# Splits of the output weights moved between slots of the last first-stage tile and chunks of the first second-stage tile

## The reference, cut to what matters

```python
scores  = scale * x @ state.T ; a  = softmax(scores)  ; xread = a  @ state   # 8 batches, 8 heads
scores2 = scale * state @ x.T ; a2 = softmax(scores2) ; sread = a2 @ x
x = concat([xread, sread])            # 8*512 + 8*32 = 4352 tokens, 512 features
h = relu(x @ w_in) ; x = (h*h) @ w_out        # first stage, width 2048
a = x @ w1 ; b = x @ w2                       # second stage, width 1024
out = ((a*b) @ w3) @ w_out2                   # computed as (a*b) @ (w3 @ w_out2)
```

## Time and profile before

| what | value |
|---|---|
| median of 3 runs | 1265.2 us (1264.62 to 1265.58) |
| profiled execution, its own time | 1264.61 us |
| its span, first to last instruction | 1263.0 us |
| PE busy | 1239.3 us (98%) |
| DVE busy | 809.8 us (64%) |
| ACT busy | 496.4 us (39%) |
| mean granted PE clock | 0.992 of full |

### The profile page before, as it was taken

How to read it: one execution, slowest core, us unless ns; L and a number is a source line. 1 busy time by engine, 2 the same in 40 slices (tenths; PEclk the granted TensorE clock), 3 DMA queues, 4 the chain that set the end, 5 groups by cost and what they waited for, 6 DMA issues and landing times.

```text
span 1263.0 us, 19633 instructions
## 1 busy us (share of the span) xinstructions
PE 1239.3 (98%) x7177; PEld 1081.5 (86%) x7177; DVE 809.8 (64%) x1445; ACT 496.4 (39%) x936; POOL 56.6 (4%) x101
## 2 busy tenths in 40 slices
PE   8988999999999999999999999999999999999998
PEld 5656888888888888888889989999999999999998
DVE  6665877678696866667544556575757575757541
ACT  6565565555555554445443412121212121212111
POOL 1000001111011100000000000000000000000000
PEclk9988999999999999999999999999999999999999
DMA  8986444444434322122112950101010110100210
GB/s 287 353 296 240 138 150 164 138 144 160 149 133 162 136 101 91 58 84 67 72 61 104 370 177 1 67 1 66 2 64 17 49 33 33 33 33 0 84 61 24
DMA packets 64632, 139.13 MB, mean 110 GB/s; under 512 B 5696, under 2 KB 6720, under 8 KB 64576
## 3 DMA queue, kind: packets, MB, share of 16 engines
q1 hardware_dynamic: 53984, 100.68, 23.7%
q0 software_dynamic: 10592, 37.75, 8.1%
HBM read 84.93 MB, written 53.48 MB: 110 GB/s over the span
## 4 chain that ended last, share of the span: by engine, by line
PE 95%; DMA 3%; DVE 1%; ACT 1%; issue 0%; SPq 0%; POOL 0%; DVEq 0%; ACTq 0%; POOLq 0%
PE ps_y L660 48%; PE ps_h L660 27%; PE ps_t L660 18%; DMA g_scratch<-g_extra 1%; DMA wp_scratch<-stage 1%; PE ps_h L719 1%; DMA g_scratch<-stage 1%; PE ps_t L719 1%; PE ps_t L684 0%; DMA raw<-in_moe_w_in 0%; DMA raw<-wp_scratch 0%; ACT GB L950 0%; DVE t L1203 0%; ACT v_hi L950 0%; DVE X_lo L1203 0%
## 5 line engine op out<-in xcount | busy, mean ns | idle before, releaser
L950 ACT CAST v_hi<-t 128x512 fp32r<-128x512 f32 (+1 forms) x216 | 129.1, 597 | 443.2 <-DVE t L1203 443.2
L660 PE MATMUL ps_y<-v_hi,X_hi 128*128 128x512 f32 (+1 forms) x576 | 219.6, 381 | 3.2 <-DVE stage L1292 3.2
L1203 DVE TENSOR_TENSOR v_lo<-t,v_hi 128x512 fp32r<-128x512 f32 (+1 forms) x216 | 143.0, 662 | 118.5 <-ACT v_hi L950 111.7
L660 PE MATMUL ps_y<-v_lo,X_hi 128*128 128x512 f32 (+1 forms) x576 | 218.2, 379 | 0.0
L660 PE MATMUL ps_y<-v_hi,X_lo 128*128 128x512 f32 (+1 forms) x576 | 218.0, 379 | 0.0
L1203 DVE TENSOR_TENSOR t<-t 128x256 f32<-128x256 f32 (+1 forms) x272 | 143.4, 547 | 103.2 <-ACT t L1050 100.2
L1050 ACT ACTIVATE t<-ps_h 128x512 f32<-128x512 f32 (+1 forms) x144 | 82.6, 573 | 158.8 <-PE ps_h L660 157.3
L660 PEld LDWEIGHTS ps_y<-v_hi,X_hi 128*128 128x128 f32 x576 | 108.7, 189 | 23.1 <-issue 3.7
L660 PEld LDWEIGHTS ps_y<-v_hi,X_lo 128*128 128x128 f32 x576 | 108.8, 189 | 20.4
L660 PEld LDWEIGHTS ps_y<-v_lo,X_hi 128*128 128x128 f32 x576 | 108.9, 189 | 19.4
L1203 DVE TENSOR_TENSOR t<-t,ps_t 128x256 f32<-128x256 f32 (+1 forms) x132 | 72.5, 549 | 48.4 <-PE ps_t L660 34.6
(11 more groups left out here) (235 smaller groups left out, 2816.9 us busy)
## 6 DMA issues: line engine op xcount, KB each, us to landing
raw<-g_scratch SPq DMA_DIRECT2D x64, 256.0 KB
raw<-in_moe_w_in SPq DMA_DIRECT2D x32, 256.0 KB
raw<-in_x_T SPq DMA_DIRECT2D x32, 256.0 KB
raw<-in_x_tok SPq DMA_DIRECT2D x32, 256.0 KB
y_scratch<-stage POOLq DMA_DIRECT2D x8, 1024.0 KB, 6.0
s_scratch<-top POOLq DMA_DIRECT2D x32, 256.0 KB, 2.5
s_scratch<-E_lo POOLq DMA_DIRECT2D x32, 256.0 KB, 3.7
raw<-y_scratch SPq DMA_DIRECT2D x8, 1024.0 KB, 5.3
```

Source lines behind the costliest of these rows:

```text
L660: mm = nc.tensor.matmul(dst, w, m, start=first and n == 0, stop=last and n == 2)
L950: return nc.scalar.copy(dst, src)
L1203: return nc.vector.tensor_tensor(dst, a, b, op)
```

## The change

Four lists change. The splits of B and the sums before them move one slot earlier or more, so that pieces of W' can stand in slots 12 to 14. Pieces 4 to 7 leave the first-stage tile: ACT rounds them, and DVE makes their low parts, at the end of chunks 1 and 2 of the second stage's tile 0. Slot 15 is empty after it.

```diff
-        set_slots = {9: [0], 10: [1], 11: [2, 3], 12: [4], 13: [5, 6]}
-        wp_slots = {14: [0, 1, 2, 3], 15: [4, 5, 6, 7]}
+        set_slots = {8: [0, 1], 9: [2, 3], 10: [4], 11: [5], 12: [6]}
+        wp_slots = {12: [0], 13: [1, 2], 14: [3]}
+        wp_chunks = {1: [4, 5], 2: [6, 7]}
...
                 copy(v_hi[:, m % 2, 0:TT], vv).then_inc(ab_hi, 1)
+                if isinstance(t, int) and t == 0:
+                    for k in wp_chunks.get(m, []):
+                        wp_round(k)
...
-                if f == 8:
+                if f == 7:
                     T_sums(0)
...
                 lower(5, 6)
+                if isinstance(t, int) and t == 0:
+                    for k in wp_chunks.get(m, []):
+                        wp_lower(k)
```

## The result

The changed kernel takes 1259.24 us (median of 6 runs, 1258.68 to 1259.9), the kernel before in the same comparison 1264.4 (6 runs, 1263.28 to 1265.58): ratio 0.996, 95% interval 0.9949 to 0.9971, which is 3.7 to 6.4 us less. The forecast was 1260.6, 4.60 us less.

A forecast was written before the change was run, and what follows sets the result against it. PE, busy 98% of the span, was taken as the bound, stalled in ab(0,0): 3.20 us of gap plus 1.40 of slow clock, 4.60 off 1264.61 gives 1260.0, or 1260.6 for the median; range 1259.4 to 1262.6.

The forecast's parts named there:

- Where the stall is and that it goes: PE waits before the fifth product of ab(0,0) for P1, behind slot 15's casts on ACT; emptying the slot gains 4.60 us.
- Rival 3: At ab(0,0), the stall stays on another wait, P1 or an operand of the fifth product: 1265.2 us, chance 0.04.
- That nothing new is late: Slots 7 to 14 and chunks 1 and 2 cost 0, at worst 0.1 us in the chunks; factor loads at ab(0,4) cost 0.
- rival 2: At ab(0,4), the last three factor loads land still later, making the kernel slower: 1268.7 us, chance 0.03.
- The step "SP": SP's loads: pieces 4 to 7 before 727 as before; later factor loads 1 to 4 us earlier, except the last three.
- the sum: Whole kernel: 1264.61 - 4.60 = 1260.0 us for the profiled execution, 1260.6 for the median, 0.36% faster.
- The price of the stall: At ab(0,0), a gap of 3.20 us before the fifth product and 1.40 us of slow clock after it, together 4.60.
- The working of the clock: Behind the gap in ab(0,0), slow matmuls cost 1.40 us by the trace, or 0.6 as an estimate, making the gain 3.8.
- The base: Whole kernel before: median 1265.2 us of the runs shown, 0.6 higher than the profiled execution's 1264.61.
- The range: Whole kernel: 1259.4 us, from a 1 us run spread, to 1262.6, with smaller clock share and short stalls at ab(0,4).
- The slots: Slots 7 to 14 of the first-stage tile: moving sums, sets and pieces 0 to 3 costs PE 0.

The follow-up runs named there:

- the run with chunk 3: The changed kernel with pieces 6 and 7 split in chunk 3 in place of 2: 1267.33 us, ratio 1.0024 to the kernel before.
- slots alone: The changed kernel with pieces 4 to 7 still split in slot 15, sums, sets and pieces 0 to 3 moved: 1264.74 us, ratio 1.0002.
- the chunks alone: The changed kernel with sums, sets and pieces 0 to 3 in their old slots, pieces 4 to 7 in chunks 1 and 2: 1259.0 us, ratio 0.9958.
- y behind alone: The kernel before with one edit of SP, pieces 4 to 7 loaded ahead of tile 1 of y: 1263.51 us, ratio 0.9992.

## Why the prediction was right and where it was wrong

- **Where the stall is and that it goes: right.** Slot 15's casts stood before P1; without them P1 is copied at +0.9 us from ab(0,0), PE needs it at +2.8, and ab(0,0) to ab(0,1) takes 7.84 us against a forecast of 729.72 - 721.90 = 7.82. Rival 3 is out.
- **That nothing new is late: right.** The sums at slot 7 and the sets in slots 8 to 12 cost nothing (PE 40.00 of 40.00), the new casts and subtractions fit in chunks 1 and 2 (0.23 us of idle time left on ACT, none on DVE), and the factor loads land about 2 us early. That they could have decided it, rival 2's mechanism, is shown by the run with chunk 3, 1.0024 of before.
- **The step "SP" had an error without effect.** I wrote "Tile 1 of y and pieces 4 to 7 are loaded before 727 as before". They are issued up to 2.7 us earlier, but in the changed kernel they land 1.5 us later against ab(0,0), the last at 727.43. Nothing waits for them there, so it cost nothing; where something waits (slots alone) their landing only 0.3 us earlier took away the whole expected gain.
- **The step that failed is the sum: both of its terms were off in size.** The sum was 1265.2 - 4.60 = 1260.6. In the comparison the kernel before took 1264.4, 0.80 us less than the first term, and the difference was 5.16 us, 0.56 more than the second; together that is the 1.36 us between 1260.6 and 1259.24. Either one alone is more than the 0.16 us by which the range was missed.
- **The price of the stall.** "3.20 us ... 1.40 us. Together 4.60" is exact for one execution and was taken for the kernel. The gap is 3.0 to 3.6 us and the clock's share 0.1 to 2.7 in five profiles of the kernel before; the timed runs put the mean sum near 5.3. The working of the clock went only to the smaller side: I gave 0.6 as the other value and let the range reach up for it, and nothing for a share above 1.40. The Trainium skill, "TensorE: Matmul & The Clock Gate", Part 1 (The HAM clock gate), says that the number of slow matmuls at the start of one kernel differs from run to run. The traces agree for a gap in mid-kernel and go further, from hardly any to about 27 of the 42 behind the gap.
- **The base.** The 1265.2 of three runs stood for a kernel whose single runs lie over 6.7 us, and "0.6 higher" than the profiled execution was carried over to the changed kernel, in which nothing corresponds to it. Without the gap its time is the start + 1138.75 + 1.6 (device time less span), so 1260.6 would need a start of 120.2, later than any in the profiles (117.87 to 120.09). The profiled execution itself, with 119.66, had one of the late starts: the 1260.0 worked out from it is right for that start, and the changed kernel's own profile, with 118.67, has 1259.05.
- **The range.** Its lower end was to be the forecast less the spread of 1 us, which is 1259.6 and not the 1259.4 given; and a spread of 1 us, from three runs, was too small.
- **The slots.** The prediction gave them no gain of their own, and none is seen: the chunks alone give 0.9958, the whole change 0.9957, and in the profiles of both everything but the start is the same to 0.1 us.

## What to carry to other kernels

When an engine that is busy for 39% of the time holds up the main one, look at what it waits for as well as at its instructions: one cast of 0.62 us left in the slot costs a gap of 1.8 us, because it waits for a load in a busy stretch. Issuing a load earlier into DMA engines that are already full need not bring it in earlier (against the start of ab(0,0): here 0.3 us earlier once, and 0.5 and 1.5 us later in two other kernels); moving its use later gave the whole gain here. And a stall of PE is not one number: take it from several executions, with the clock behind it, before a range is made from it. Nor is what is left without the stall: here the start alone differs by 2.2 us. The change that removes the stall also narrows the spread, from 6.3 us (35 runs) to 1.4 (12, the changed kernel and the chunks alone) on the same chip.

## What the hardware showed that I had not expected

- Among gaps of 2.9 to 3.6 us, the length alone does not decide whether the clock falls. It fell after gaps of 2.92, 3.20, 3.45, 3.56 and 3.61 us and not after 3.02 and 3.39 (in the same place; kernel before, slots alone, y behind alone); not after 1.67 and 1.78 in one profile each. When it fell, it stood at 0.50, 1.2 GHz, and cost between 1.4 and 2.7 us; when not, 0.1.
- Loads of one queue can slow or pass each other: a piece of 256 KB issued 0.36 us before 1 MB of y landed 4.99 us after its issue, and the first piece, issued 1.74 us ahead of it, landed 4.18 us ahead, 2.5 us after its issue. In the stretch around 746, with little else in the engines, the same size lands in 2.5 to 3.6 us (changed kernel and chunks alone).
- The start of the program, the same code in all kernels, takes 117.9 to 120.1 us up to the steady part, and that is most of the spread of the changed kernel. What sets it was not tried.
